# One half of batch 0's attention moves from VectorE to TensorE, and 12 instead of 18 weight tiles are split first

## The reference

```python
# attention, per batch and head: a pooled part and a band
q_d, k_d, v_d = (x.reshape(B, H, Sd, 4, D).mean(axis=3) for x in (q, k, v))   # Sd = 144
out_up = np.repeat(sm_attn(q_d, k_d, v_d), 4, axis=2)
mask = np.abs(pos[:, None] - pos[None, :]) < 4          # a band of 7 keys for each token
scores = np.where(mask, scale * q @ k.T, -1e9)
x = out_up + softmax(scores) @ v                        # -> (2304, 512)
# first MLP, 512 -> 2048 -> 512
h = np.maximum(x @ w_in, 0.0); x = (h * h) @ w_out
# second MLP, 512 -> 3 x 768, maximum of the three -> 512
h = np.maximum(np.maximum(x @ w1, x @ w2), x @ w3); out = h @ w_out2
```

## Time and profile before

| | |
|---|---|
| median of 3 runs | 842.93 us (842.84 to 844.95) |
| the profiled execution | 842.53 us, span of its trace 840.8 us |
| PE busy | 808.3 us (96%) |
| DVE busy | 486.3 us (58%) |
| ACT busy | 329.7 us (39%) |
| POOL busy | 238.7 us (28%) |
| PE up to 20 us, 20 to 40 us | 11.0, 18.4 us busy |
| first matmul of `up(0)` | at 56.28 us |

### The profile page before, as it was taken

One profiled execution on the slowest core, in us unless ns is written; L12 is line 12 of the kernel. 1 busy time (PEld: TensorE's weight loads), 2 busy tenths in 40 slices (PEclk: granted clock), 3 DMA queues, 4 the chain that ended last, 5 costly groups with the idle time before them and its releaser, 6 DMA issues.

```text
span 840.8 us, 13445 instructions
## 1 busy us (share of the span) xinstructions
PE 808.3 (96%) x5548; PEld 779.9 (93%) x5548; DVE 486.3 (58%) x552; ACT 329.7 (39%) x852; POOL 238.7 (28%) x205
## 2 busy tenths in 40 slices
PE   5979979999999999999999999999999999999996
PEld 5779978989999999999999999999999999999996
DVE  5979996899978999778970028522221213122212
ACT  3665555454575455654544343221212112121111
POOL 1899933244612364323444223000000000000000
PEclk9999989999999999999999999999999999999999
DMA  9942240012410044100000055310111102010001
GB/s 216 320 137 62 50 116 17 5 40 66 123 34 25 16 94 122 29 23 22 1 30 1 1 166 153 111 42 0 39 38 37 40 1 76 1 38 0 19 20 38
DMA packets 41892, 49.75 MB, mean 59 GB/s; under 512 B 11496, under 2 KB 33000, under 8 KB 40936
## 3 DMA queue, kind: packets, MB, share of 16 engines
q1 hardware_dynamic: 41264, 48.08, 21.0%
q10 hardware_dynamic: 568, 0.82, 0.4%
HBM read 37.39 MB, written 10.62 MB: 57 GB/s over the span
## 4 chain that ended last, share of the span: by engine, by line
PE 83%; DVE 7%; ACT 4%; POOL 3%; issue 1%; DMA 1%; SPq 0%; ACTq 0%; DVEq 0%
PE PS L531 25%; PE PS L533 25%; PE PS L532 24%; DVE sc L982 2%; DVE tmp L972 2%; PE PS L571 2%; PE PS L591 2%; PE PS L669 2%; POOL G L1317 1%; PE PS L561 1%; ACT x L827 1%; POOL XS L1296 1%; PE PS L579 1%; DMA qk<-q 1%; ACT qkT L787 1%
## 5 line engine op out<-in xcount | busy, mean ns | idle before, releaser
L531 PE MATMUL PS<-XS,WI 128*128 128x288 f32 (+1 forms) x768 | 243.1, 317 | 1.2 <-ACT G L842 1.2
L532 PE MATMUL PS<-XS,WI 128*128 128x288 f32 (+1 forms) x768 | 238.9, 311 | 0.0
L533 PE MATMUL PS<-XS,WI 128*128 128x288 f32 (+1 forms) x768 | 238.7, 311 | 0.0
L1317 POOL TENSOR_TENSOR G<-g,G 128x288 fp32r<-128x288 f32 x128 | 150.4, 1176 | 253.5 <-ACT G L842 253.2
L531 PE MATMUL PS<-G,WO 128*128 128x288 f32 x512 | 156.7, 306 | 1.0 <-POOL G L1317 1.0
L532 PE MATMUL PS<-G,WO 128*128 128x288 f32 x512 | 151.6, 296 | 0.0
L533 PE MATMUL PS<-G,WO 128*128 128x288 f32 x512 | 151.4, 296 | 0.0
L531 PEld LDWEIGHTS PS<-XS,WI 128*128 128x128 f32 x768 | 145.1, 189 | 5.1 <-issue 1.9
L532 PEld LDWEIGHTS PS<-XS,WI 128*128 128x128 f32 x768 | 145.6, 190 | 1.3
L533 PEld LDWEIGHTS PS<-XS,WI 128*128 128x128 f32 x768 | 145.3, 189 | 0.0
L835 ACT ACTIVATE PS<-PS 128x288 f32<-128x288 f32 x128 | 50.8, 397 | 156.8 <-PE PS L533 140.1
(11 more groups left out here) (139 smaller groups left out, 1180.3 us busy)
## 6 DMA issues: line engine op xcount, KB each, us to landing
vb<-v SPq DMA_DIRECT2D x4, 1152.0 KB, 8.0
x_scratch<-x2s SPq DMA_DIRECT2D x8, 576.0 KB, 3.5
XR<-x_scratch SPq DMA_DIRECT2D x6, 768.0 KB, 4.9
qk<-q SPq DMA_DIRECT2D x7, 576.0 KB, 5.3
out<-osb SPq DMA_DIRECT2D x15, 256.0 KB
qk<-k SPq DMA_DIRECT2D x3, 1152.0 KB, 7.7
WIr<-moe_w_in SPq DMA_DIRECT2D x3, 1024.0 KB, 15.8
WOr<-moe_w_out SPq DMA_DIRECT2D x3, 1024.0 KB, 15.1
```

Source lines behind the costliest of these rows:

```text
L531: mm(dst, wt(HI), xt_(HI), start=first, stop=False)
L532: mm(dst, wt(HI), xt_(LO), start=False, stop=False)
L533: return mm(dst, wt(LO), xt_(HI), start=False, stop=last)
L1317: Q.tensor_tensor(G[:, s % NGR, LO], g32[:, s % 2], G[:, s % NGR, HI].bitcast(f32), ALU.subtract).then_inc(g_ready, 1)
```

## The change

Batch 0 is cut otherwise. Its first 288 tokens (`HT`), in natural order, are chunk 0; the other 288 tokens are chunk 1, in 16 groups of 18 rows, and only they are DVE's.

- **First half on PE.** Three blocks of 96 tokens (`QR`), each with 104 keys (`KR`). q and k are loaded by token, four tokens to a partition, one DMA a head (256-byte pieces), and transposed two heads at a time (`features`). `block_scores` does 8 products for each block (96 x 104) and adds a large number outside the band by 8 transposes of `unseen`; DVE takes the minimum (`block_lows`), ACT the exponential (`block_exps`, one for each head), PE turns the probabilities (`block_probs`), DVE copies them out (`block_turned`), PE multiplies with v and a column of ones (`block_outputs`), DVE divides (`block_normed`). The pooled attention of these tokens goes the same way for two groups of four heads, and `first_block` adds both in PSUM, from where ACT and DVE make the high and low parts.
- **Pooled attention of the other half** moves behind the opening: its s, t and o tasks are woven in steps 1 to 6 of chunk 0 (`HEADS_AT[0]`), each with half the products.
- **Second half.** As before on DVE, but the scores are in `sc` (SBUF) for every n. Its x tasks stand 1.5 steps earlier, at (0, 13, 0) to (0, 14, 2); the tasks of the other batches stand 1 to 3 steps earlier.
- **Weights.** 12 tiles are split ahead, in the order 0 to 7, 8, 10, 12, 9. The other 20 follow in steps 0 to 12 of chunk 0, alternately two and one a step. w_in and w_out from block 8 on are loaded once the scratch in their place is free, which is after the opening's last product.
- The sums of v for the pooled part move from POOL to DVE (`pool_first_v`); `keep_busy`, the cleared accumulators and `add_weighted` are gone.
- `out_moves` stores the first 288 tokens in natural order.

The core of the diff:

```diff
-    W_AHEAD, W_BEFORE_X = 18, 16
+    W_ORDER = list(range(8)) + sorted(range(8, NW1), key=lambda i: (i // 2 + LAG * (i % 2), -i))
+    W_AHEAD = 12
+    W_LATE, left = [], W_ORDER[W_AHEAD:]
+    while left:
+        W_LATE.append([left.pop(0) for _ in range(min(len(left), 2 - len(W_LATE) % 2))])
     def w_late(s):
-        return [W_AHEAD + s] if W_AHEAD + s < NW1 else []
+        return W_LATE[s] if s < len(W_LATE) else []
...
+    opening = [(kind, c) for c in range(KC) for kind in ("qT", "kT")]
+    opening += [("qP", 0), ("kP", 0)] + pair("S", 0) + [("kP", 1)] + pair("S", 1) + pair("ps", 0) + pair("P", 0)
+    opening += pair("S", 2) + pair("ps", 1) + pair("O", 0) + pair("P", 1) + pair("pt", 0)
+    opening += pair("O", 1) + pair("P", 2) + [("po", 0)] + pair("pt", 1) + pair("O", 2) + [("po", 1)]
+    firsts = [("first", i) for i in range(BL)] + [("qP", 1)]
...
-    QK_AT = {1: (1, 1, 2), 2: (2, 13, 1), 3: (4, 10, 2)}
-    HEADS_AT = {1: (1, 3, 2), 2: (2, 15, 3), 3: (4, 13, 1)}
-    X_AT = {0: [None, None, None, (0, 14, 2), (0, 14, 3), (0, 15, 0)],
-            1: [(1, 14, 1), (1, 14, 3), (1, 15, 1), (2, 8, 3), (2, 9, 2), (2, 10, 0)],
+    QK_AT = {1: (1, 0, 2), 2: (2, 10, 2), 3: (4, 7, 2)}
+    HEADS_AT = {0: (0, 1, 0), 1: (1, 2, 2), 2: (2, 13, 0), 3: (4, 10, 1)}
+    X_AT = {0: [None, None, None, (0, 13, 0), (0, 13, 3), (0, 14, 2)],
+            1: [(1, 12, 1), (1, 12, 3), (1, 13, 1), (2, 6, 2), (2, 7, 1), (2, 7, 3)],
...
-    EXP_AT = {(0, 6): 1, (2, 0): 3, (3, 12): 5, (5, 10): 7}
+    EXP_AT = {(0, 5): 1, (1, 15): 3, (3, 11): 5, (5, 8): 7}
...
-        def scores_of(n):
-            return PS[:, (3, 7)[n], :HR * BAND].rearrange("p (i o) -> p i o", o=BAND) if n < 2 else sc[:]
```

SP's queue:

```diff
+            for h in range(NH):
+                sp.dma_start(TOK[:UNITS, 0, 0, :, h], q[0][h, :HT, :].rearrange("(p t) d -> p t d", t=POOL)).then_inc(q_pair_loaded[h // 2], 16)
+            load_tok(1, k, k_tok_loaded)
+            sp.wait_ge(zeroed, 1)
...
+            load_w_in(0)
+            load_w_out(0)
...
+            sp.dma_start(qk[:, HR:GL, :], half_groups(q, HT, S)).then_inc(q_loaded[1], 16)
+            load_half("k", k, k_loaded)
+            load_w_in(1)
+            load_w_out(1)
+            load_tok(0, q, q_tok_loaded)
+            load_w_in(2)
+            load_w_out(2)
+            load_half("v", v, v_loaded)
+            filled(sp, 0, firsts[-1])
+            for n in (3, 4):
                 load_w_in(n)
                 load_w_out(n)
```

ACT's queue of the opening:

```diff
+            for c in range(KC):
+                q_features(c)
+            pooled_q_features(0)
+            for i in range(2):
+                for e in range(2):
+                    block_exps(i, e)
+            for e in range(2):
+                pooled_exps(0, e)
+            split_next(2)
+            for e in range(2):
+                block_exps(2, e)
+            split_next(2)
+            for e in range(2):
+                pooled_exps(1, e)
+            split_next(2)
+            for e in range(2):
+                pooled_turned(0, e)
+            split_next(2)
+            for e in range(2):
+                pooled_turned(1, e)
+            split_next(2)
+            for i in range(BL):
+                ps = bank(("first", i))
+                A(first_x(i, HI), view(ps[:, :KC * QR], "p (c q) -> p c q", c=KC), ACT.Copy).then_inc(first_hi[i], 1)
+            pooled_q_features(1)
+            split_next(W_AHEAD)
```

DVE's, from the last operations of the opening into chunk 0:

```diff
+            pool_first_v()
...
+            seg = score_steps(1, three)
+            run(seg, 1)
+            block_normed(1)
+            block_turned(2)
+            run(seg, 1)
+            pooled_normed(0)
+            block_normed(2)
+            pooled_normed(1)
+            for i in range(BL):
+                run(seg, 1)
+                first_lo_part(i)
+            for h in range(NH):
+                run(seg, 1)
                 head_max(0, h)
```

More of the change, by code:

```diff
@@ new lines, in bank, with full, two_heads, features @@
+                return PS[:, ATT[bk]]
+            def full(ins, task):
+                ins.then_inc(att_full[bank_of(0, task)], 1)
+            def two_heads(x, c, t):
+                return view(x[:, t, 2 * c:2 * c + 2], "p h d -> p (h d)")
+            def features(which, c):
+                task = (("qT", "kT")[which], c)
+                ps, cnt = bank(task), UNITS + which
+                pe.wait_ge((q_pair_loaded, k_pair_loaded)[which][c], 32)
+                for t in range(POOL):
+                    last = nc.tensor.transpose(ps[:, cnt * t:cnt * (t + 1)], two_heads(TOK[:cnt, which, 0], c, t), ident[:cnt, :cnt])
+                full(last, task)
@@ new lines, in pooled_features @@
+            def pooled_features(which, n):
+                task = (("qP", "kP")[which], n)
+                ps = bank(task)
+                if n:
+                    pe.wait_ge((q_tok_loaded, k_tok_loaded)[which], 16 * POOL)
+                else:
+                    for loaded in (q_pair_loaded, k_pair_loaded)[which]:
+                        pe.wait_ge(loaded, 32)
+                for c in range(KC):
+                    for t in range(POOL):
+                        last = mm(ps[:, UNITS * c:UNITS * (c + 1)], two_heads(TOK[:UNITS, which, n], c, t), ident[:UNITS, :UNITS],
+                                  start=t == 0, stop=t == POOL - 1, is_transpose=True)
+                full(last, task)
@@ new lines, in pooled_scores @@
+            def pooled_scores(a):
+                ps = [bank(task) for task in pair("ps", a)]
+                for t in (("qP", 0), ("kP", 0), ("kP", 1)):
+                    read(pe, 0, t)
+                for i in range(2):
+                    last = [mm(ps[e][:SB, SD * i:SD * (i + 1)], qkT[64 * e:64 * e + 64, 0, 2 * a + i, q_part(0)],
+                               qkT[64 * e:64 * e + 64, 1, 2 * a + i, :], start=True, stop=True) for e in range(2)]
+                for e in range(2):
+                    full(last[e], ("ps", a, e))
@@ new lines, in first_block @@
+            def first_block(i):
+                ps = bank(("first", i))
+                for e in range(2):
+                    read(pe, 0, ("O", i, e))
+                    read(pe, 0, ("po", e))
+                pe.wait_ge(spread_made, 3)
+                for c in range(KC):
+                    at, f = slice(QR * c, QR * (c + 1)), slice(P * c, P * (c + 1))
+                    mm(ps[:, at], out_first[i][:, f], ident[:QR, :QR], start=True, stop=False, is_transpose=True)
+                    last = mm(ps[:, at], od_first[:, f], spread[:, QR * i:QR * (i + 1)], start=False, stop=True)
+                full(last, ("first", i))
```

740 lines of the change are left out of this document (378 added, 362 removed), and 4 rows, old and new, of the table X_AT.

## The result

The changed kernel took **947.49 us** (median of 4 runs, 944.91 to 948.79) beside 842.88 for the kernel before: a ratio of 1.1232, with a 95% interval of 1.1202 to 1.1262. The forecast was 846.5, in a range of 836 to 855. The direction was the one with the largest chance, and the time was off by 101 us. The profiled execution has a span of 943.4 us, against 840.8.

What follows compares the result with a forecast made beforehand. The prediction took the time as the opening, PE's work, and PE's losses in chunk 0 and at chunk 1's start. 842.5 less 8.3 gained plus 12 lost gave 846.2, 846.5 us for the median; range 836 to 855.

Steps and rivals of the forecast that it cites:

- there at about 9 us: Opening: the last pair of q and k, 16 DMAs and 1.19 MB, loaded by about 9 us.
- U = 48: End of the opening: U, the start of `up(0)`, at 48 us against 56.3, 8.3 us gained; bounds 45 to 54.
- My 1.6 us for the clock: Opening: 1.6 us added because PE's idle time costs clock.
- the opening gains little: Rival, opening: small-piece loads and PE's slow clock bring U to 54; 852 us, chance 0.11.
- The heads, 6.2 us: Chunk 0: eight pooled-attention heads with half their products, moved behind U, take PE 6.2 us.
- Each waits for a whole operation of the other, in turn: Chunk 0: POOL and DVE alternate waits, 11 us; DVE's half 1 done at U + 56, 10 later than before.
- lines 1044 and 1056 at 1.9 to 2.4 us: Sign in chunk 0: DVE's operations of half 1 at these two lines last 1.9 to 2.4 us each.
- U + 68: Start of chunk 1: `up(16)` starts 68 us behind U, against U + 52.9 before.
- What I expected back inside chunk 1, 3 us: Chunk 1: the 2.1 us wait inside `up(16)` and some slow clock behind it go, giving back 3 us.
- Moved places, costed at nothing: Batches 1 to 3: moved places keep their distance to DVE's work, cost nothing; if DVE is late, each makes PE wait.
- SP's queue: Behind U: late loads reach tile 16 at U + 5, ACT needs it at U + 7; cover 2 us.
- the waits stay small: Rival, chunk 0: POOL and DVE seldom collide, half 1 done at U + 47; 839 us, chance 0.32.

Runs made afterwards that it cites:

- experiment 1: The changed kernel with ACT's eight loads of k by token going to 80 partitions instead of 73; 880.97 us, ratio 1.0452.
- experiments 1 and 2: The second of these: the changed kernel with ACT's loads of k in 74 partitions instead of 73; 922.38 us, measured once.
- 8: Changed kernel with 80 partitions, two identity transposes before opening tasks, v's sums on POOL, DVE pausing in half 1's value steps, old places of batches 1 to 3; 862.80 us.
- 9: On top of 8, weight tiles 0 to 15 split ahead in place of 12; 861.09 us, ratio 1.0194.
- experiment 6: On top of experiment 1, the sums of v for the pooled part back on POOL, ahead of its first tile; 877.28 us, ratio 1.0403.
- the fillers: On top of experiment 1, four unused transposes of the identity before each of PE's opening tasks except the first-block ones; 875.93 us, ratio 1.0388.
- experiment 4: On top of experiment 1, DVE waits for the end of each value-step operation of half 1 before sending the next; 880.46 us, ratio 1.0449.
- experiment 10: On top of 8, POOL's 20 late low parts cut short, ACT filling the rest with raw weights (products not exact); 859.53 us, ratio 1.0188.
- experiment 7: On top of experiment 1, the places of batches 1 to 3 as in the kernel before; 869.69 us, ratio 1.0312.
- 11: On top of experiment 1, POOL's late low parts cut short, ACT filling the rest with raw weights; 880.70 us, ratio 1.0436.

## Why the prediction was wrong, point by point

**The last pair of q and k "there at about 9 us": this step failed, and it is 66 of the 101 us.** I priced the 16 DMAs by their bytes at the GB/s of the earlier trace rows and by the rate of 256-byte pieces of the earlier trace rows. Both rows are of loads of other shapes. q came nearly as forecast, its last pair at 10.5 us in experiment 1. k, in 73 partitions, came at 76.5 us, with ACT's sequencer standing in line 989 until 70.6 (experiments 1 and 2): alone it moved 71 packets of 256 bytes a us, 18 GB/s, where I had taken over 200. The trace of before has no load of such a shape, and I didn't mark the price as unknown, so no bound of the range held it. What follows is read for the opening in experiment 1, where this step is mended, and for the chunks in the changed kernel.

**U = 48: still 17 us too early.** In experiment 1 it is 65.3, outside my bounds of 45 to 54.
- *Small products of PE.* I took 2.6 us for a score block, 1.2 for a `first_block` and 1.3 for the outputs of a block. From one start to the next they take 4.4, 2.4 and 2.6. From 10.5 us to U, 54.8 us, the chain of experiment 1 is PE's own work but for 5.0. The loads of the tiles, on which I had hung a part of U, are not on it. My durations were those of the higher level of the clock, as this instruction in three kernels says (shortest/median/longest in ns). In 8 it runs at a granted clock of 0.50 (1.2 GHz):

```profile
L727 PE MATMUL PS<-prs,x x24: 421/421/422, 48.7 to 55.4; 72*128 72x96 f32 x24
```

In the changed kernel, in a window that reads 1.00:

```profile
L725 PE MATMUL PS<-prs,x x24: 421/421/422, 122.1 to 128.7; 72*128 72x96 f32 x24
```

```profile
124.00:129.00 5.00, 5.00 (x28) 5.00 (x28) 3.45 (x4) 0.98 (x2) 0.00 (x0) 1.00 0.02 3
```

In 9, in a window at 1.00 as well:

```profile
L727 PE MATMUL PS<-prs,x x24: 272/275/275, 51.3 to 54.8; 72*128 72x96 f32 x24
```

The two readings of 1.00 are not the same thing. The first record of the clock in a trace stands where it rises for the first time: at 11.8 us in the kernel before, 10.1 in 8, 33.7 in 9, 133.3 in the changed kernel. What lies ahead has no record and prints 1.00. The timeline of PE in 9 shows the rise, four products of a score block before and after it:

```profile
28.42 0.66 PE L664 MATMUL PS<-WIr 64*96 64x104 f32 x4
...
34.26 0.42 PE L664 MATMUL PS<-WIr 64*96 64x104 f32 x4
```

So PE was at the lower level all through the opening of the changed kernel and of experiment 1 (first record at 68.9), and some us into `up(0)`. Behind the rise of 9 a score block takes 2.6 us, a `first_block` 1.24 and a block's outputs 1.3, just what I had taken. My 1.6 us for the clock should have been about 13: 5.3 for three score blocks, 3.4 for `first_block`, 4.0 for the outputs. The rival "the opening gains little" had this mechanism, at 1.3 times my durations where it was 1.7 to 2.0. The kernel before rose 3 us after its first transpose, amid 72 of them in a row, and had `keep_busy` behind them; the changed kernel has neither, and these runs don't say which of the two it lacked.
- *DVE's sums of v* (lines 1273 to 1275) stood in front of the divisions: 5.2 us (experiment 6). In the changed kernel they take 8.1 us, beside POOL's tiles; I had not priced them. With the 11 us by which the clock was too cheap this makes 16 of the 17; how far the two overlap isn't shown.
- What the fillers buy they nearly cost: U is 61.6 with them, and with all the mends together 57.9 (8) or, with 16 tiles ahead as well, 56.1 (9), where it was before. The gain of 8.3 us is not there in any version.

**The heads, 6.2 us.** In chunk 0 their three lines are 3.7, 3.6 and 2.4 us busy: 9.7, counted with some overlap. The term was mis-sized by up to 3.5.

**"Each waits for a whole operation of the other, in turn": the mechanism failed, the sum was too small.** Half 1 is done at U + 52.6 (forecast U + 56), and "lines 1044 and 1056 at 1.9 to 2.4 us" is not what the trace shows for nine steps in a row: 1.34. In these DVE lost nothing; one operation of POOL lasted 12.3 us in place of 0.8, PE waited 9.8 for it, and from 174.3 to 184.5 the granted clock was 0.50. Where DVE is made to pause (experiment 4), the turns are there as forecast, 1.83 to 2.34, and PE waits less in all; the chunk is still 73.1 long. `up(16)` was to start at U + 68 and started at U + 76.1: from the end of half 1 to there it is 23.5 us, not my 12, since PE was behind by then. What I expected back inside chunk 1, 3 us, came: 2.5.

Chunk 0 in rows, with the columns of the earlier trace rows, before:

```profile
56.30:109.20 52.90, 50.66 (x370) 50.23 (x370) 52.09 (x44) 29.67 (x76) 50.57 (x34) 0.97 0.28 63
```

after:

```profile
130.80:206.90 76.10, 62.40 (x436) 57.63 (x435) 57.03 (x54) 39.28 (x109) 67.16 (x40) 0.93 0.42 115
```

experiment 10:

```profile
60.00:129.70 69.70, 62.63 (x436) 57.89 (x435) 50.66 (x52) 50.23 (x131) 49.33 (x41) 0.94 0.46 125
```

Of the 23.2 us that chunk 0 grew by, PE is busy for 11.7 more (62.40 less 50.66: the heads, and matmuls at the lower clock) and idle for 11.5 more (13.7 less 2.2); its waits for G are 11.9 of the 13.7. In experiment 10, with about 17 us less for POOL to do, PE is still busy for 62.6 and idle for 7.1. So POOL's and DVE's common work is only a part. The rest is the heads in the chunk, their waits for ACT, and stretches at the lower clock, of which in 10 the first 5.2 us are the opening's (0.50 up to 65.2). I forecast 15.1 us for chunk 0 (U + 68 against U + 52.9) and got 23.2; how much of the rest is each one's, these runs don't separate.

**Moved places, costed at nothing: 11 us in experiment 7.** I wrote that each would be a wait of PE if DVE were late. DVE was: PE's waits for it are 6.1 and 5.2 us, and chunks 2 and 4 are 7.1 and 9.2 us longer, of which the neighbouring chunks give back 2.5 to 6.7. The sentence was right and the price should not have been zero: the tasks had been moved 1 to 3 steps earlier, and DVE's half 1 ended 7 us later behind U than before. My own forecast had it 10 later, so the waits followed from it.

**SP's queue** (2 us of cover): behind U the lists of waits show none of PE for a weight tile and none of ACT for a load; right.

**The direction** was right, in part by luck: the largest loss is the load of k, where I had seen none, and the opening never gained. What remains of my reasons is that chunk 0 loses more than the opening can give: with the one number mended the kernel is 4.5% slower, with all mends 2.3%, and with 16 tiles as well 1.9%. The rival on the other side, "the waits stay small", was clearly wrong: it had chunks 0 and 1 grow by 4 us together, and they grew by 20.7. No version here beats the kernel before. (Two sums of the prediction are off by little, which changes nothing here: U + 44.7 with 16 waits of 1.06 is U + 61.7, not 61, and the rival's 842.9 - 2.3 + 12 is 852.6, not 852. The step of the load of tiles goes from 31 us and under 1 more to 33 without saying by what.)

The sum, in spans: opening 82.8 above the forecast (65.5 k, 17.3 the rest), chunk 0 8.1, chunk 1 0.5, all that follows 7.3; together 98.7, and 2 more between span and median.

## What to carry to other kernels

Look at the partition count of every new load before its bytes: 73 instead of 80 cost 66 us here, and rows of loads of other shapes had no sign of it. Before you price small matmuls, take their durations from a stretch that is as sparse as the new one will be; if the nearest row is of a full stretch, the other level is a bound of the range. Compare one instruction's duration in two stretches before you believe the column of the clock. And where a row shows that two engines hold each other up, a row of operations without a pause on one can hold the other for all of it, so ask which of them will be sent back to back, and what is queued behind the one that stands.

## What the runs showed of the hardware

- **The number of partitions of a load.** 73, 74 and 80: landed at 76.5, 51.2 and under 11 us, and the issuing engine's sequencer was held for 69.8, 31.8 and 6.2 us; in the changed kernel ACT's first instruction of its own comes at 70.6. With 73 the load moved 18 GB/s when nothing else moved.
- **A shut-out in both directions.** POOL's operation of 0.8 us lasted 12.32 us behind nine of DVE's with two inputs in SBUF, to the hundredth the same in the changed kernel and in 11; DVE's of 1.34 us lasted 8.18 behind POOL's tiles. The Trainium skill (SBUF — State Buffer, "SBUF: two separate sides") says that whichever starts first holds the shared ports for the whole instruction and the other fully blocks. The turns in the earlier trace rows and in experiment 4 agree; the two long stands go beyond it, since they last over a row of instructions.
- **A granted clock of 1.00 is no proof of the 2.4 GHz level where the trace has no record of the clock.** The same product took 421 ns in a window at 0.50, 421 ns in one that prints 1.00 ahead of the first record (133.3 us), and 275 ns in one at 1.00 behind it (33.7 us in 9).
- **A wait can cost the clock behind it.** In experiment 9 waits of 2.8 us between 60 and 65 us were followed by a granted clock of 0.50 from 64.4 to 74.7, in which PE did 24 matmuls in six microseconds in place of 46.
